# Attention scores of two heads in the two row halves of TensorE, one shared load and split of q and k, and another order of the engines' work

## What is computed

```
scores = q @ k^T / 8                        # [4, 8, 576, 576]
cum = cumsum(log(clip(f, 1e-4, 1)))
scores = where(causal, -1e9, scores + cum[q] - cum[k])
attn = exp(scores - max); attn /= sum + 1e-9
x = attn @ v                                # as [2304, 512]
x = x / rms(x) * g
x = (silu(x @ w_gate) * (x @ w_val)) @ w_out        # width 1536
out = silu(x @ w_in) @ w_out2                       # width 2048
```

## Time and profile before

| | us |
|---|---|
| median of 3 runs | 1099.25 |
| lowest, highest | 1098.27, 1100.86 |
| the profiled execution | 1097.32 |
| its span, first to last instruction | 1095.4 |

### The profile page before, as it was taken

How to read it: one execution, slowest core, us unless ns; L and a number is a source line. 1 busy time by engine, 2 the same in 40 slices (tenths; PEclk the granted TensorE clock), 3 DMA queues, 4 the chain that set the end, 5 groups by cost and what they waited for, 6 DMA issues and landing times.

```text
span 1095.4 us, 17477 instructions
## 1 busy us (share of the span) xinstructions
PE 1050.4 (96%) x6094; PEld 959.5 (88%) x6094; DVE 365.8 (33%) x835; ACT 378.7 (35%) x835; POOL 288.4 (26%) x323
## 2 busy tenths in 40 slices
PE   4998989889999999999999999999999999999998
PEld 3666666679999999999999999899999899999997
DVE  3666666653623224124223223221211212111111
ACT  4667777733213113123132121222223223232222
POOL 5877777637701102002000278400000000000000
PEclk9999999999999999999999999999999999999999
DMA  8877787403200000000000133100000000000000
GB/s 204 229 217 217 210 216 193 122 1 98 77 0 0 0 0 0 0 0 0 0 0 0 31 104 106 49 1 29 0 0 29 0 29 0 0 29 0 29 1 29
DMA packets 34428, 61.55 MB, mean 56 GB/s; under 512 B 4880, under 2 KB 8976, under 8 KB 34384
## 3 DMA queue, kind: packets, MB, share of 16 engines
q1 hardware_dynamic: 34384, 60.99, 20.0%
HBM read 56.17 MB, written 4.79 MB: 56 GB/s over the span
## 4 chain that ended last, share of the span: by engine, by line
PE 82%; DMA 4%; POOL 3%; DVE 3%; issue 3%; ACT 3%; SPq 1%; POOLq 0%; DVEq 0%; ACTq 0%
PE banks L945 17%; PE banks L947 17%; PE banks L946 17%; PE banks L1030 6%; PE banks L1031 6%; PE banks L1029 6%; PE banks L901 4%; DMA w_stage<-w 4%; PE banks L869 3%; ACT qk_hi L528 1%; POOL w_main L442 1%; DVE ptb L677 1%; PE banks L842 1%; PE banks L843 1%; DVE probs L667 1%
## 5 line engine op out<-in xcount | busy, mean ns | idle before, releaser
L945 PE MATMUL banks<-xn,w_main 128*128 (+1 forms) x504 | 169.7, 337 | 2.9 <-POOL w_kept L442 1.6
L947 PE MATMUL banks<-xn,w_main 128*128 (+1 forms) x504 | 169.6, 337 | 0.0
L946 PE MATMUL banks<-xn,w_main 128*128 (+1 forms) x504 | 169.3, 336 | 0.0
L947 PE MATMUL banks<-xn,w_kept 128*128 (+1 forms) x408 | 136.8, 335 | 0.0
L945 PE MATMUL banks<-xn,w_kept 128*128 (+1 forms) x408 | 136.7, 335 | 0.0
L946 PE MATMUL banks<-xn,w_kept 128*128 (+1 forms) x408 | 136.6, 335 | 0.0
L768 DVE TENSOR_TENSOR gated_sb<-banks,act_sb 128x384 f32<-128x384 f32 x72 | 40.1, 556 | 228.6 <-PE banks L947 205.5
L521 ACT ACTIVATE probs<-probs,row_min 128x128 f32<-128x128 f32 (+2 forms) x144 | 83.7, 581 | 54.9 <-DVE row_min L667 54.7
L945 PEld LDWEIGHTS banks<-xn,w_main 128*128 128x128 f32 x504 | 94.9, 188 | 6.1 <-issue 3.4
L946 PEld LDWEIGHTS banks<-xn,w_main 128*128 128x128 f32 x504 | 94.9, 188 | 2.3
L947 PEld LDWEIGHTS banks<-xn,w_main 128*128 128x128 f32 x504 | 95.0, 188 | 0.0
(11 more groups left out here) (147 smaller groups left out, 2161.1 us busy)
## 6 DMA issues: line engine op xcount, KB each, us to landing
w_stage<-w SPq DMA_DIRECT2D x68, 256.0 KB, 2.7
qk_raw<-qk_t SPq DMA_DIRECT2D x64, 144.0 KB, 3.2
cum_b<-cum_dram SPq DMA_DIRECT2D x32, 288.0 KB, 5.0
qk_raw<-qk_t SPq DMA_DIRECT2D x32, 160.0 KB, 3.2
v_sb<-v_p SPq DMA_DIRECT2D x16, 320.0 KB, 4.4
cum_t<-cum_dram SPq DMA_DIRECT2D x32, 144.0 KB, 5.2
out<-out_sb SPq DMA_DIRECT2D x18, 256.0 KB, 2.1
qk_raw<-qk_t SPq DMA_DIRECT2D x32, 128.0 KB, 3.3
```

Source lines behind the costliest of these rows:

```text
L945: nc.tensor.matmul(dst, w_hi_part, m_hi, start=start, stop=False)
L946: nc.tensor.matmul(dst, w_hi_part, m_lo, start=False, stop=False)
L947: return nc.tensor.matmul(dst, w_lo_part, m_hi, start=False, stop=stop)
```

## The change

`scores` takes a whole group: both heads at once. q and k of head 0 stand in partitions 0 to 63, those of head 1 in 64 to 127, so a matmul of head 0 uses the upper 64 rows of the array and one of head 1 the lower 64, each into a bank of its own; three products (hi hi, lo hi, hi lo) in place of four. The tail gets a copy of the last 64 queries with zeros beside it and three matmuls for each half in place of four. Groups alternate between banks 0, 1 and 2, 3. q and k are loaded once (three DMAs a pair), into one buffer `qk_raw` in place of one for each head, rounded by DVE in one instruction of 1280 columns and split by POOL in one. The loops run over pairs: PE does the transposes of tiles 2 to 8 of a pair, and its values, in the iteration of the next pair, between the score groups. DVE's and ACT's order and the share of copies (`BY_ACT`) change with it; "r1" goes to DVE. POOL spreads the row factors behind the second weight piece. 20 pieces of weights are split in pairs 0 to 9, in place of 18 in pairs 0 to 11.

```diff
+GROUPS = NFULL + 1
+Q_AT, K_AT, REST_AT = 0, SEQ, 2 * SEQ
+QK_COLS = 2 * SEQ + 2 * REST
-BY_ACT = frozenset((0, 1, "t1", "r0", "r1"))
+BY_ACT = frozenset((1, 3, 4, 6, "t0", "r0"))
-MAIN = 18
+MAIN = 20
+W_OF_PAIR = [range(2 * p, 2 * p + 2) if 2 * p < MAIN else range(0) for p in range(NPAIRS)]
+SQUARES_PAIR, MEAN_PAIR = 10, 14
...
-        qk_raw = sb("qk_raw", [P, 2, 2 * SEQ], F32, att)
+        qk_raw = sb("qk_raw", [P, QK_COLS], F32, att)
...
+        def score_bank(p, g):
+            return 2 * ((GROUPS * p + g) % 2)
...
+            def load_qk(p):
+                wait(sp, qk_split, p)
+                sp.dma_start(qk_raw[:, 0:2 * SEQ],
+                             qk_t[2 * p:2 * p + 2].rearrange("a d two s -> (a d) (two s)")).then_inc(qk_in, 16)
+                for hh in range(2):
+                    sp.dma_start(qk_raw[hh * DH:(hh + 1) * DH, REST_AT + hh * REST:REST_AT + (hh + 1) * REST],
+                                 qk_t[2 * p + hh:2 * p + hh + 1, :, 0, SEQ - REST:SEQ].rearrange("a d s -> (a d) s")
+                                 ).then_inc(qk_in, 16)
...
-            def split_qk(p, hh):
+            def split_qk(p):
...
+                pool.wait_ge(qk_hi_done, p + 1)
+                nc.gpsimd.tensor_tensor(qk_lo[:, b, :], qk_raw[:, :], f32(qk_hi[:, b, :]),
                                         ALU.subtract).then_inc(qk_split, 1)
...
             for p in range(NPAIRS):
                 if p + 1 < NPAIRS:
+                    split_qk(p + 1)
+                for n in W_OF_PAIR[p][0:1]:
                     split_weight(n // 2, n % 2, w_piece(n, 0), w_piece(n, 1))
+                row_sums(p)
+                for n in W_OF_PAIR[p][1:2]:
+                    split_weight(n // 2, n % 2, w_piece(n, 0), w_piece(n, 1))
+                spread_factors(p)
...
+            for s in range(3):
+                exps(0, s)
+            for p in range(NPAIRS + 1):
+                here, following = p < NPAIRS, p + 1 < NPAIRS
+                if here:
+                    take_out(p, 1)
+                    exps(p, 3)
+                    exps(p, 4)
+                else:
+                    for c in range(DC):
+                        xn_hi(0, c)
+                if p > 0:
+                    row_scales(p - 1)
+                if here:
+                    exps(p, 5)
+                    exps(p, 6)
+                    take_out(p, 3)
+                    exps(p, 7)
+                    take_out(p, 4)
+                    exps(p, 8)
+                    take_out(p, 6)
+                if following:
+                    exps(p + 1, 0)
+                    exps(p + 1, 1)
+                if p == MEAN_PAIR:
+                    first_guess(0)
+                if here:
+                    take_out(p, "t0")
+                if following:
+                    exps(p + 1, 2)
...
+            def qk_round(p):
+                dve.wait_ge(qk_in, 48 * (p + 1))
+                wait(dve, scored, TILES * (p - 1))
+                nc.vector.tensor_copy(qk_hi[:, p % 2, :], qk_raw[:, :]).then_inc(qk_hi_done, 1)
...
+            for p in range(NPAIRS + 1):
+                here, following = p < NPAIRS, p + 1 < NPAIRS
+                if here:
+                    shift(p, 3)
+                if p > 0:
+                    take_out(p - 1, 7)
+                if p > 1:
+                    x_out(p - 2, 1)
+                if p > 0:
+                    take_out(p - 1, "t1")
+                if here:
+                    shift(p, 4)
+                else:
+                    xn_lo(0, 0)
...
+                if p > 0:
+                    invert(p - 1)
+                if following:
+                    qk_round(p + 1)
...
+                if here:
+                    take_out(p, 0)
+                    shift(p, 5)
+                    shift(p, 6)
+                if p > 0:
+                    row_scales(p - 1)
+                if here:
+                    shift(p, 7)
+                    take_out(p, 2)
+                    shift(p, 8)
+                if following:
+                    shift(p + 1, 0)
+                if p > 0:
+                    x_out(p - 1, 0)
+                if here:
+                    take_out(p, 5)
+                if following:
+                    shift(p + 1, 1)
+                    shift(p + 1, 2)
+                if p == MEAN_PAIR + 1:
+                    for c in range(DC):
+                        normalise_x(0, c)
...
+            def scores(p, g):
                 b = p % 2
+                if g == 0:
+                    pe.wait_ge(qk_split, p + 1)
+                if GROUPS * p + g >= 2:
+                    pair, group = divmod(GROUPS * p + g - 2, GROUPS)
+                    pe.wait_ge(shifted, TILES * pair + min(2 * group + 2, TILES))
...
+                if g < NFULL:
+                    cols = max(WIDTH[g], 192)
...
+                    for n, (q, k) in enumerate(((hi, hi), (lo, hi), (hi, lo))):
+                        for hh in range(2):
+                            head = slice(hh * DH, (hh + 1) * DH)
+                            nc.tensor.matmul(banks[:, bank + hh, 0:cols], q[head, query], k[head, keys],
+                                             start=(n == 0), stop=False)
+                    for hh in range(2):
+                        nc.tensor.matmul(banks[:, bank + hh, P * g:P * (g + 1)], ident_bf, mask_bf[:, :],
+                                         start=False, stop=True).then_inc(scored, 1)
...
             for p in range(NPAIRS):
+                if p > 0:
+                    both(p - 1, 1)
+                if p > 1:
+                    values(p - 2, 1, (2, 3, 4))
+                scores(p, 0)
+                if p > 0:
+                    both(p - 1, 2)
+                scores(p, 1)
+                if p > 0:
+                    both(p - 1, 3)
+                scores(p, 2)
+                if p == MEAN_PAIR:
+                    first_mean()
+                if p > 0:
+                    transposes(p - 1, TAIL, "t0", range(NFULL))
+                    transposes(p - 1, TAIL, "t1", range(NFULL, NT))
+                scores(p, 3)
+                both(p, 0)
...
+                if p > 0:
+                    values(p - 1, 0, (0, 1))
+                    values(p - 1, 1, (0, 1))
+                    row_factors(p - 1)
+                scores(p, 4)
...
+            both(NPAIRS - 1, 1)
+            values(NPAIRS - 2, 1, (2, 3, 4))
+            both(NPAIRS - 1, 2)
+            both(NPAIRS - 1, 3)
+            transposes(NPAIRS - 1, TAIL, "t0", range(NFULL))
+            transposes(NPAIRS - 1, TAIL, "t1", range(NFULL, NT))
             pe.wait_ge(shifted, TILES * NPAIRS)
             up(0, 0, 0)
+            values(NPAIRS - 1, 0, (0, 1))
+            values(NPAIRS - 1, 1, (0, 1))
             row_factors(NPAIRS - 1)
+            values(NPAIRS - 1, 1, (2, 3, 4))
             up(0, 0, 1)
```

More of the change, by code:

```diff
@@ L173, in build @@
         scanned = sem("scanned")
-        qk_in = [sem(f"qk_in{h}") for h in range(2)]
+        qk_in = sem("qk_in")
         cum_in = [sem(f"cum_in{b}") for b in range(2)]
@@ L330, in load_weight @@
                 sp.dma_start(w_stage[:, slot, :], src).then_inc(w_in[slot], 16)
-            def load_qk(p, hh):
-                wait(sp, qk_split, 4 * (p - 1) + 2 * hh + 2)
-                source = qk_t[2 * p + hh:2 * p + hh + 1].rearrange("a d two s -> (a d) (two s)")
-                for half in range(2):
-                    for here, there in raw_columns(hh):
-                        sp.dma_start(qk_raw[half * DH:(half + 1) * DH, hh, there], source[:, here]).then_inc(qk_in[hh], 16)
+            def load_qk(p):
[6 more added lines that the diff above has]
+                                 ).then_inc(qk_in, 16)
             def load_cum(p):
@@ L522, in exps @@
                                      accum_out=row_sum[:, p % 2, s:s + 1]).then_inc(exped, 1)
-            def qk_round(p, hh):
-                act.wait_ge(qk_in[hh], 64 * (p + 1))
-                wait(act, scored, TILES * (p - 1))
-                nc.scalar.activation(qk_of(p % 2, hh), qk_raw[:, hh], ACT.Copy).then_inc(qk_hi_done, 1)
             def take_out(p, entry):
@@ L713, in normalise_x, with xn_lo @@
                                                op0=ALU.mult, op1=ALU.mult).then_inc(x_normed, 1)
+            def xn_lo(t, tiles_before):
+                for c in range(DC):
+                    dve.wait_ge(xn_hi_done, DC * (t + tiles_before) + c + 1)
+                    nc.vector.tensor_tensor(xn_of(t, 1, c), x_sb[:, c, tokens(t)], f32(xn_of(t, 0, c)),
+                                            ALU.subtract).then_inc(xn_split, 1)
             dve.wait_ge(gain_in, 16)
-            for s in range(AHEAD_SHIFT):
+            qk_round(0)
@@ L717, in _ @@
+            for s in range(3):
                 shift(0, s)
-            for p in range(NPAIRS):
-                for s in range(TILES):
-                    if ahead(p, s, AHEAD_SHIFT):
-                        shift(*ahead(p, s, AHEAD_SHIFT))
```

(30 more changed lines are left out.)

170 lines of the change are left out of this document (42 added, 128 removed).

## The result

The changed kernel takes 1074.0 us (median of 4 runs, 1072.28 to 1074.47) against 1099.15 us (median of 4): 0.9767 of the time before, 95% interval 0.975 to 0.9783, 25 us less. Forecast were 1070 and a range of 1058 to 1088.

A forecast was written before the change was run, and what follows sets the result against it. PE was taken as nearest to the bound, in the part before 238 us: 1.8 us a pair less over 15 pairs, 27.0, and 2 at the ends give 29 us, so 1099.25 to 1070; 8 in 10 range 1058 to 1088.

The forecast's parts named there:

- The total: Whole kernel: 15 pairs x 1.8 us and 2 us at the two ends, 29 us less, median from 1099.25 to 1070.
- The bound: PE is nearest to full, 11.85 of a pair's 13.12 us; the feed-forward part, 857 us, isn't touched.
- The stalls: PE's waits for banks that ACT and DVE empty late, about 1.8 us a pair: nearly all go, 0.3 left.
- PE's work: PE's own work in a pair: 11.3 + 0.1 (groups) - 0.26 (tail) - 0.15 (values) = 11.0 us.
- rival 1: Loads of the two row halves overlap too: PE's work 10.3 us a pair, 1060 us in all; chance 0.12.
- the visit of the values: PE's change of array shape at the values, 0.05 + 0.10 = 0.15 us, taken as the price for each group.
- `qk_round` on DVE: Rounding of 1280 columns of q and k on DVE, taken as 0.9 us; cover of 1 to 1.5 us.
- the upper bound of 4.4: Longest `qk_round` on DVE, at the rate of a 384-column instruction that took 1.33 us while POOL worked.
- The start: Ahead of the pairs: `cum_dram` issued behind three DMAs in place of eight, 1.1 us earlier; a third lost to filling.
- Pair 14: Pair with ACT's table loads ahead of the copy of t0: 2.2 us longer than others again, 1 more at worst.
- "Other things of this part ... cost nothing.": Rest of the attention part, and two more weight pieces (1.9 us of POOL each, in idle time), add no time.
- The rule of the Trainium skill: PE's weight loads take columns divided by 1.2 GHz whatever the rows: 107 ns for 128, six loads 0.64 us a group.

The follow-up runs named there:

- split_twice: The changed kernel with POOL's subtraction of 1280 columns done twice, first into an unread buffer: 1121.07 us against 1097.36 of the kernel before.
- full_rows_two: The changed kernel with four score matmuls over all 128 rows in a full group, eight in the tail; wrong attention, for timing: 1070.47 us, 10.97 a pair.
- full_rows: The changed kernel with each of a full group's six score matmuls over all 128 rows; wrong attention, for timing: 1088.04 us, 11.97 a pair.
- by_head: The changed kernel with the three score matmuls of head 0 ahead of the three of head 1: 1076.61 us, 11.04 a pair.

## Why the prediction was right, point by point

- **The total.** 1074 for 1070 is in part luck. The ten steady pairs gained 3.1 us more than forecast (21.1 for 18), the last five 9.5 less (0.5 lost, for 9.0 gained), and 2.4 us come from where the two profiled executions lie beside their medians.
- **The bound.** PE as the bound and the feed-forward part unmoved: right.
- **The stalls.** That 1.8 us a pair would go, and that no other wait would come: right. PE stands for nothing between 31 and 141 us. The split on POOL as the tightest place, with 1 us in hand: right; POOL's loop has the split at 2.93 us (forecast 2.9 to 3.1), and in `split_twice` as much again made the pairs at full clock 1.9 us longer, so 1.0 was in hand.
- **PE's work.** 11.0 us forecast for it, and 11.02 measured, but the 0.3 us left for late semaphores weren't needed, and errors met. The two loads of a pass cost nothing beside its stream (rival 1 was right there: four groups take 3.2 us in place of 4.0), and a visit costs 0.28 to 0.33 us in place of 0.15. That step failed by the row that it took: the visit of the values was counted from its first matmul, while the way in stands ahead of it, in the transposes (0.76 for six, 0.58 over full rows). With the ways in counted, the row halves cost the four groups 0.3 us more than four full-row matmuls each (3.2 + 0.53 for 3.4), where the forecast had 0.1. What made up for it is the base: the forecast had 11.3 - 0.15 = 11.15 us for the old matmuls in the new order, and `full_rows_two` shows 10.97, so the old order had cost 0.2 us a pair more than the 1.8 counted.
- **`qk_round` on DVE.** 0.9 forecast, 0.77 measured; the upper bound of 4.4 never came. What POOL paid (1.09 for 0.61) I hadn't priced.
- **The start.** 1.1 us forecast from `cum_dram`. It was issued at 5.95 us in place of 7.12, but the first shift started at 14.04 in place of 16.26, 2.2 us earlier. The write also landed sooner: SP issued the first read of it at 7.62 us (before 9.38), 1.8 us earlier. The last 0.5 are sooner landings of the reads. That fewer DMAs stood beside these loads is a guess.
- **Pair 14.** 2.2 us more than a steady one forecast, at worst 3.2; 13.88 - 11.02 = 2.9 measured. The forecast calls PE half idle at the hand-over; its own row has PE busy for 6.67 of 8.00 us.
- **"Other things of this part ... cost nothing."** The step that failed. The squares moved from pair 12 to pair 10, and in POOL's queue from a place ahead of `row_sums` to one behind the spread. My own laying out had POOL's loop with 1 us in hand; 2.8 and 5.6 us (140.20 to 142.97, 154.53 to 160.11) of new work inside that loop could not be hidden. I listed the loop for steady pairs and didn't lay out the special ones. It cost 9.8 us in the pairs; with it moved, the time is 1065.7, 4 below the forecast.
- **The rule of the Trainium skill** on loads: the profile shows passes of 192 columns in 0.11 us for both heads together (122.28 to 122.39 above), so two loads of 128 columns passed in 0.11 us. Timeline of the loads (PEld) of the first pass of group 0, in the changed kernel and in `full_rows`:

```profile
122.09 0.19 PEld L849 LDWEIGHTS banks<-qk_hi 64*128 64x128 f32 x2
```

```profile
106.66 0.30 PEld L848 LDWEIGHTS banks<-qk_hi 128*128 128x128 f32 x2
```

  Both loads of the row halves fit in the 0.19 us of one; over full rows the second starts 0.11 us after the first. So the loads of the two halves run at the same time. By the Trainium skill's page "TensorE: Matmul & The Clock Gate", section on LDWEIGHTS, each would take 107 ns, and two in a row 214, an estimate from that page; they don't stand in a row here. Part 3 of the same page of the Trainium skill, on packing small matmuls, says that a load overlaps with matmuls in flight if its rows differ from theirs; the overlap of the halves is of that kind, and it is what I should have weighed beside the first rule. Its "only when" the rows differ is too narrow for this trace, though: in `full_rows` the second load of a 512-column pass runs from 100.16 to 100.35 us, beside a matmul of the same rows that started at 100.16. A load of 64 rows seems no shorter than one of 128: at 192 columns a pass of the halves follows the last by 0.11 us and a matmul over full rows by the same 0.11 (0.22 for two, 106.97 to 107.19 in `full_rows`), where the stream alone would need 0.08. The Trainium skill's page "TensorEngine Tiling (Array Packing)", section Tiling Modes, says that a change of the tiling mode drains the engine; these rows show 0.18 us on the way in and 0.10 on the way out.

## What to carry to other kernels

Lay out the queue of each engine once for the steady iteration and once for each special one: an engine with a loop of waits through it (here spread, split, scores) has no idle time to give, even when it is busy for 4.7 us of 11. When a long instruction is moved in a queue, count what stands behind it: the same rounding cost 0.88 us a pair in one place of ACT's queue and nothing in another. Row halves are worth what they save in copies, loads and splits of operands; on the matrix engine itself, with visits of three passes, they only broke even, and the visits should be long.

## What the runs showed of the hardware

- Matmuls in the two row halves start together (within 0.010 us) even if three of the one half stand ahead of those of the other in the program (11.04 against 11.03 us a pair). Their loads run at the same time too. The Trainium skill's page "TensorE: Matmul & The Clock Gate", Part 2, says that matmuls stay in program order and that only loads are pulled ahead. Where two row halves are in use, the start times of `by_head` differ from that, and the measurement decides.
- A change between 64-row and 128-row matmuls took 0.18 us on the way in and 0.10 on the way out; four more visits cost 1.32 us. A part of it shows as longer transposes ahead, not at the matmuls themselves.
- A spread on POOL took 1.09 us beside a rounding of 0.77 us on DVE, and 0.61 without.
- After stalls of 1.7 and 4.5 us PE's granted clock was 0.88 and 0.80 in the mean of the pair; after the same stall of 2.6 us it was 1.00 in one kernel and 0.81 in another, and with a stall of 1.9 us in every pair it was 1.00 and 0.88 in turn.
